# An attention and two-MLP kernel: the second MLP's Gelu writes back into its PSUM bank, and the cast and the subtraction read the bank instead of an SBUF tile

## The chip, the cores and the metric

The kernel runs on one core of one Trainium2 chip. The metric is device time in microseconds; it is given as the median of several runs. A profile is one execution recorded by the hardware profiler.

## The reference, cut to what matters

```python
# attention: q (1, 12288, 128); kv (1, 384, 32, 128), pooled over 4x4 windows -> 768 keys
kv_flat = kv_pool.reshape(B, -1, C) @ w_sr          # keys = values
a = softmax(q @ kv_flat.T / sqrt(C))
x = a @ kv_flat                                     # (12288, 128)
# first MLP, d_ff = 2048
h = x @ w_in;  g = maximum(h, 0) + alpha * minimum(h, 0);  y = g @ w_out
# second MLP, d_ff = 2048
h = y @ w_in2; g = h * (1 / (1 + exp(-1.702 * h)));        out = g @ w_out2
```

All arrays are float32. The second MLP's activation is the sigmoid form of Gelu, which ScalarE computes in one instruction (Gelu_apprx_sigmoid).

## The kernel before, in words

The tokens are cut into 24 tiles of 512 (TILES = 24, TOK = 512). The features (128) lie on the partitions, the tokens along the free dimension. Each product is done in float32r as three matmuls on operands that are split into a high part (a cast to float32r) and a low part (the exact value minus the high part): high x high, high x low, low x high (`passes`, L713 to L715, and L758, L761, L762 in `up`).

Each MLP has 2048 hidden features, in CH = 16 chunks of 128, numbered f. For every chunk:

- `up(t, m, f)` on TensorE (PE): three matmuls into bank f % 4 of the PSUM tile ps_h (RING = 4);
- first MLP (m = 0): `relu_hi` on ScalarE (ACT, L436) writes g_hi out of ps_h, and `relu_lo` on VectorE (DVE, L606) writes g_lo = relu(ps_h) - g_hi. Both read the bank;
- second MLP (m = 1): `gelu` on ACT (L440) reads ps_h and writes the SBUF tile g_full. The cast g_full to g_hi is made by ACT (L444) for odd f (CAST_ON_ACT) and by DVE (L614) for even f. `gelu_parts` on DVE then writes g_lo = g_full - g_hi (L616);
- `down(t, m, f)` on PE: three matmuls of g_hi and g_lo into ps_y1 or ps_y2. It waits on the semaphore g_split, which L606 and L616 increment.

PE runs `down(f - 3)` behind `up(f)` (LAG = 3). `up(f + 4)`, which fills the bank of f again, has no wait of its own: it stands behind `down(f)` in PE's order. In the second MLP of tile t the attention scores of tile t + 1 stand between up and down at f = 2, 4, 5, 7, 8 and 10 (SCORES_AT, ps_s); ACT copies them to s_sb (L419), DVE keeps a running maximum over them (`chunk_max`, L554), and behind f = 11 (MAX_AT) comes `token_max` (L560 to L580), which finds the maximum over the keys for each token and hands it to a DMA that spreads it over the partitions (max_row, max_sb). At f = 4 there is the split of the attention output (`attended_lo`, L621) and at f = 6 the inverse of the softmax's denominators (`inverse_sums`, L560 to L595). GpSimd (POOL) subtracts the maximum from the scores (L339) and sums the exponentials (L353). The first MLP of tile t holds the exponentials of tile t + 1 and the product with the values.

All orders are written out by hand, the same for each tile: tile 0, a hardware loop over tiles 1 to 21, then tile 22 (no scores and no maxima) and tile 23 (no attention at all). Every engine waits only on semaphores; a same-engine dependency has its own (act_done, dve_cast).

At the start g_full also serves as the place of the transposed first weight (w_in1T_sb), which one DMA of ACT's queue fills and which PE reads before the first Gelu (L824).

Of the kernel before, what the change touches and what calls it, by code (L numbers as in the profile page):

```python
# [11 lines left out]
P = 128  # L12
POOL = 4
WINDOW = POOL * POOL
TOK = 512
BLOCKS = TOK // P
LAG = 3
RING = 4
# [7 lines left out]
def attention_mlp_kernel(  # L26
# [14 lines left out]
    FF = w_in1.shape[1]  # L41
# [32 lines left out]
    with ExitStack() as ctx:  # L74
        def sb(name, shape, dt=F32):
            return ctx.enter_context(nc.sbuf_tensor(name, shape, dt))

        def psum(name, shape):
            return ctx.enter_context(nc.psum_tensor(name, shape, F32))

        def sem(name):
            return ctx.enter_context(nc.semaphore(name))

        ps_h = psum("ps_h", [P, RING, 512])
# [32 lines left out]
        y_lo = sb("y_lo", [P, TOK], F32R)  # L117
        g_hi = sb("g_hi", [P, RING, TOK], F32R)
        g_lo = sb("g_lo", [P, RING, TOK], F32R)
        g_full = sb("g_full", [P, RING, TOK])  # L120
        out_sb = sb("out_sb", [P, TOK])

        kv_raw = sb("kv_raw", [P, KV_RING, KV_KEYS, WINDOW])
# [16 lines left out]
        warm = sb("warm", [P, 1])  # L140
        warm_out = sb("warm_out", [P, 1])


        w_raw2 = kv_raw[:].rearrange("p r k w -> p (r k w)")
        w_in1T_sb = g_full[:].rearrange("p r n -> p (r n)")


        q0_raw, q0_hi, q0_lo = y_full, y_hi, y_lo
# [62 lines left out]
        act_cast = sem("act_cast")  # L211
        dve_cast = sem("dve_cast")
# [8 lines left out]
        def f32(ap):  # L221
            return ap.bitcast(F32)
# [27 lines left out]
        def casts_before(f, on_act):  # L250
            return sum((j in CAST_ON_ACT) == on_act for j in range(f))
# [141 lines left out]
        def _(act):  # L393
# [43 lines left out]

            def gelu(t, f):
                act.wait_ge(up_done, t * UPS + (CH + f + 1))
                nc.scalar.activation(g_full[:, f % RING, :], ps_h[:, f % RING, :],  # L440
                                     ACT.Gelu_apprx_sigmoid).then_inc(act_done, 1)
                if f in CAST_ON_ACT:
                    act.wait_ge(act_done, t * UPS + (CH + f + 1))
                    nc.scalar.copy(g_hi[:, f % RING, :], g_full[:, f % RING, :]).then_inc(act_cast, 1)  # L444

            def attended_hi(u):
                act.wait_ge(attended, u * KC + KC)
# [8 lines left out]
            def tile(t, attend, score):  # L456
                for f in range(LAG, CH):
                    relu_hi(t, f)
                    if attend and f in EXP_AT:
                        exponentials(t + 1, EXP_AT[f], t)  # L460
                        exponentials_hi(t + 1, EXP_AT[f])
                    if first(t) and f in W2_HI_AT:
                        second_hi(W2_HI_AT[f])
                nc.scalar.activation(warm_out[:], warm[:], ACT.Gelu_apprx_sigmoid)

                for f in range(CH):
                    gelu(t, f)
                    if score and f in SCORES_AT:
                        scores_to_sbuf(t + 1, SCORES_AT[f])
                    if attend and f == ATTENDED_AT:  # L470
                        attended_hi(t + 1)
                if attend:
                    nc.scalar.activation(warm_out[:], warm[:], ACT.Exp)
                    for f in range(LAG):
                        relu_hi(t + 1, f)

                act.wait_ge(y_complete, t * 2 + 2)
                if not first(t):
                    act.wait_ge(out_stored, t * DMA)
                nc.scalar.copy(out_sb[:], ps_y2[:]).then_inc(out_made, 1)  # L480
# [36 lines left out]
        def _(dve):  # L517
# [91 lines left out]
            def gelu_parts(t, f):  # L609
                if f in CAST_ON_ACT:  # L610
                    dve.wait_ge(act_cast, t * CASTS_ACT + (casts_before(f, True) + 1))
                else:
                    dve.wait_ge(act_done, t * UPS + (CH + f + 1))
                    nc.vector.tensor_copy(g_hi[:, f % RING, :], g_full[:, f % RING, :]).then_inc(dve_cast, 1)  # L614
                    dve.wait_ge(dve_cast, t * CASTS_DVE + (casts_before(f, False) + 1))
                nc.vector.tensor_tensor(g_lo[:, f % RING, :], g_full[:, f % RING, :], f32(g_hi[:, f % RING, :]),  # L616
                                        ALU.subtract).then_inc(g_split, 1)

            def attended_lo(u):
# [12 lines left out]
            def tile(t, attend, score):  # L632
                for f in range(LAG, CH):
                    relu_lo(t, f)
                    if score and f == QUERIES_AT:
                        queries_hi(t + 1)
                    if first(t) and f == FIRST_SUMS_AT:
                        inverse_sums(0)
                    if attend and f in LO_AT:
                        weights_lo(t + 1, LO_AT[f])  # L640
                for c in range(len(LO_AT), KC if attend else 0):
                    weights_lo(t + 1, c)

                divide(t)
                for f in range(CH):
                    gelu_parts(t, f)
                    if attend and f == ATTENDED_AT:
                        attended_lo(t + 1)
                    if attend and f == SUMS_AT:
                        inverse_sums(t + 1)  # L650
                    if score and SCORES_AT.get(f, 0) >= 1:
                        chunk_max(t + 1, SCORES_AT[f])
                    if score and f == MAX_AT:
                        token_max(t + 1)
                if attend:
                    for f in range(LAG):
                        relu_lo(t + 1, f)
# [211 lines left out]
```

## Time and profile before

| | |
|---|---|
| median of 3 runs | 1328.65 us (1327.99 to 1331.34) |
| profiled execution | 1329.05 us |
| its span in the profile | 1327.2 us, so 1.85 us lie around it |
| TensorE busy | 1288.1 us (97%) |
| VectorE busy | 992.1 us (75%) |
| ScalarE busy | 909.8 us (69%) |
| GpSimd busy | 409.5 us (31%) |
| mean granted TensorE clock | 0.993 of full speed |

The page gives busy time for each engine. Matmuls overlap in the engine, so a matmul's duration (about 390 ns) is longer than the distance from one start to the next (about 230 ns in the steady stretches). The times of DVE and ACT instructions overlap a little too: the next one can start before the record of the last one ends. The chain of work that ended last follows each instruction back to what released it.

### The profile page before, as it was taken

To read this page: it belongs to the slowest core of one execution; us is meant where nothing else is said; L and a number is where in the kernel's file an instruction comes from. 1 tells how busy PE (TensorE), PEld (TensorE's weight loads), DVE (VectorE), ACT (ScalarE), POOL (GpSimd) and SP (SyncE) were. 2 spreads that over 40 slices of the span, in tenths; PEclk is the share of its full clock that TensorE was granted. 3 is DMA by queue.
4 is the path that set the end of the run, shared out by engine and by line. 5 is a ranking of instruction groups with operands and counts; after the bars stand their busy time and mean duration, and the time that the engine had idled before them with its cause. 6 is when DMAs were issued, how large, how long until landed. Compare 5 with 4: busy or idle time off the path is not lost.

```text
span 1327.2 us, 18973 instructions
## 1 busy us (share of the span) xinstructions
PE 1288.1 (97%) x5608; PEld 1046.1 (79%) x5608; DVE 992.1 (75%) x1759; ACT 909.8 (69%) x1570; POOL 409.5 (31%) x305
## 2 busy tenths in 40 slices
PE   5689999999999999999999999999999999999998
PEld 3478888888888888888888888888888888888886
DVE  6997867768678677687786776877867768778665
ACT  3567667776776667767766677677666776776665
POOL 1773142241331422413314224133042241340400
PEclk9799999999999999999999999999999999999999
DMA  8201000000010000000100000000001000000000
GB/s 283 100 17 32 9 24 24 14 26 20 12 32 8 24 24 16 24 24 8 32 8 24 26 14 24 24 8 32 9 22 29 10 24 24 8 24 12 13 16 8
DMA packets 17935, 36.81 MB, mean 28 GB/s; under 512 B 3456, under 2 KB 3584, under 8 KB 17280
## 3 DMA queue, kind: packets, MB, share of 16 engines
q1 hardware_dynamic: 17488, 33.47, 7.8%
q10 hardware_dynamic: 432, 3.15, 0.6%
q8 instruction: 8, 0.13, 0.0%
q14 instruction: 7, 0.06, 0.0%
HBM read 30.22 MB, written 6.39 MB: 28 GB/s over the span
## 4 chain that ended last, share of the span: by engine, by line
PE 86%; DVE 10%; ACT 3%; issue 1%; DMA 1%; SPq 0%; POOL 0%; DVEq 0%; ACTq 0%
PE ps_y L713 13%; PE ps_y L714 12%; PE ps_y L715 12%; PE ps_h L761 12%; PE ps_h L762 12%; PE ps_h L758 11%; PE ps_x L713 2%; DVE g_lo L616 2%; PE ps_x L715 2%; PE ps_x L714 2%; PE ps_s L713 2%; PE ps_s L715 2%; PE ps_s L714 2%; DVE parts_max L562 1%; DVE pooled L560 1%; ACT g_full L440 1%
## 5 line engine op out<-in xcount | busy, mean ns | idle before, releaser
L606 DVE SCALAR_TENSOR_TENSOR g_lo<-ps_h,g_hi 128x512 fp32r<-128x512 f32 x384 | 262.8, 690 | 207.3 <-ACT g_hi L436 204.8
L339 POOL TENSOR_TENSOR s_sb<-s_sb,max_sb 128x512 f32<-128x512 f32 x138 | 174.5, 1301 | 655.2 <-DMA max_sb<-max_row 655.2
L440 ACT ACTIVATE g_full<-ps_h 128x512 f32<-128x512 f32 x384 | 229.7, 599 | 192.5 <-PE ps_h L762 181.5
L436 ACT ACTIVATE g_hi<-ps_h 128x512 fp32r<-128x512 f32 x384 | 227.1, 596 | 157.6 <-PE ps_h L762 157.1
L713 PE MATMUL ps_y<-g_hi,down_hi 128*128 128x512 f32 x768 | 302.1, 393 | 6.1 <-DVE g_lo L606 2.9
L714 PE MATMUL ps_y<-g_lo,down_hi 128*128 128x512 f32 x768 | 299.2, 390 | 0.0
L715 PE MATMUL ps_y<-g_hi,down_lo 128*128 128x512 f32 x768 | 299.1, 389 | 0.0
L616 DVE TENSOR_TENSOR g_lo<-g_full,g_hi 128x512 fp32r<-128x512 f32 x384 | 260.0, 688 | 38.3 <-ACT g_hi L444 31.7
L713 PEld LDWEIGHTS ps_y<-g_hi,down_hi 128*128 128x128 f32 x768 | 144.1, 188 | 46.6 <-DVE g_lo L616 12.4
L353 POOL TENSOR_TENSOR exp_sum<-exp_sum,s_sb 128x512 f32<-128x512 f32 x92 | 140.2, 1524 | 91.9 <-ACT s_sb L426 91.4
L715 PEld LDWEIGHTS ps_y<-g_hi,down_lo 128*128 128x128 f32 x768 | 144.2, 188 | 30.4
L714 PEld LDWEIGHTS ps_y<-g_lo,down_hi 128*128 128x128 f32 x768 | 144.2, 188 | 28.9
L761 PE MATMUL ps_h<-y_lo,up_hi 128*128 128x512 f32 x384 | 151.3, 394 | 0.9 <-DVE y_lo L630 0.9
L758 PE MATMUL ps_h<-y_hi,up_hi 128*128 128x512 f32 x384 | 149.6, 390 | 1.2 <-DVE y_hi L628 1.2
L758 PE MATMUL ps_h<-x_hi,up_hi 128*128 128x512 f32 x384 | 149.7, 390 | 0.0
L762 PE MATMUL ps_h<-y_hi,up_lo 128*128 128x512 f32 x384 | 149.7, 390 | 0.0
L761 PE MATMUL ps_h<-x_lo,up_hi 128*128 128x512 f32 x384 | 149.6, 390 | 0.0
L762 PE MATMUL ps_h<-x_hi,up_lo 128*128 128x512 f32 x384 | 149.4, 389 | 0.0
L444 ACT CAST g_hi<-g_full 128x512 fp32r<-128x512 f32 x192 | 119.4, 622 | 6.1
L601 DVE TENSOR_TENSOR a_lo<-s_sb,a_hi 128x512 fp32r<-128x512 f32 x138 | 113.0, 819 | 10.6 <-ACT a_hi L432 10.6
L614 DVE CAST g_hi<-g_full 128x512 fp32r<-128x512 f32 x192 | 81.2, 423 | 37.3 <-ACT g_full L440 35.2
L432 ACT CAST a_hi<-s_sb 128x512 fp32r<-128x512 f32 x138 | 86.0, 623 | 4.4
(142 smaller groups left out, 1714.4 us busy)
## 6 DMA issues: line engine op xcount, KB each, us to landing
kv_raw<-kvT SPq DMA_DIRECT2D x12, 512.0 KB, 5.5
inv_sb<-inv_row SPq DMA_DIRECT2D x24, 256.0 KB, 3.0
outT<-out_sb SPq DMA_DIRECT2D x24, 256.0 KB, 2.0
q_raw<-qT SPq DMA_DIRECT2D x23, 256.0 KB, 2.7
max_sb<-max_row SPq DMA_DIRECT2D x23, 256.0 KB, 3.1
w_raw<-w_in SPq DMA_DIRECT2D x1, 1024.0 KB, 8.0
w_raw<-w_out SPq DMA_DIRECT2D x1, 1024.0 KB, 9.9
g_full<-w_in1T ACTq DMA_DIRECT2D x1, 1024.0 KB, 5.2
```

Source lines behind the costliest of these rows:

```text
L339: nc.gpsimd.tensor_tensor(s_sb[:, c, :], s_sb[:, c, :], max_sb[:], ALU.subtract).then_inc(diff_done, 1)
L353: nc.gpsimd.tensor_tensor(exp_sum[:], (scores_of(u, 0) if c == 1 else exp_sum[:]), scores_of(u, c), ALU.add).then_inc(exp_sum_done, 1)
L436: nc.scalar.activation(g_hi[:, f % RING, :], ps_h[:, f % RING, :], ACT.Relu).then_inc(act_done, 1)
L440: nc.scalar.activation(g_full[:, f % RING, :], ps_h[:, f % RING, :], ACT.Gelu_apprx_sigmoid).then_inc(act_done, 1)
L606: nc.vector.scalar_tensor_tensor(g_lo[:, f % RING, :], ps_h[:, f % RING, :], 0.0, f32(g_hi[:, f % RING, :]), ALU.max, ALU.subtract).then_i ...
L616: nc.vector.tensor_tensor(g_lo[:, f % RING, :], g_full[:, f % RING, :], f32(g_hi[:, f % RING, :]), ALU.subtract).then_inc(g_split, 1)
L713: nc.tensor.matmul(out, w_hi_ap, m_hi_ap, start=start, stop=False)
L714: nc.tensor.matmul(out, w_hi_ap, m_lo_ap, start=False, stop=False)
L715: return nc.tensor.matmul(out, w_lo_ap, m_hi_ap, start=False, stop=stop)
L758: nc.tensor.matmul(ps_h[:, f % RING, :], up_hi[m][:, cols(f)], src_hi[:], start=True, stop=False)
L761: nc.tensor.matmul(ps_h[:, f % RING, :], up_hi[m][:, cols(f)], src_lo[:], start=False, stop=False)
L762: nc.tensor.matmul(ps_h[:, f % RING, :], up_lo[m][:, cols(f)], src_hi[:], start=False, stop=True).then_inc(up_done, 1)
```

## The change

Gelu writes its result back into the bank of ps_h from which it reads. The cast on ACT, the cast on DVE and DVE's subtraction read that bank. The SBUF tile g_full is given up, and w_in1T_sb gets a tile of its own of the same size. Semaphores, orders and loops stay as they are.

```diff
-        g_full = sb("g_full", [P, RING, TOK])
...
-        w_in1T_sb = g_full[:].rearrange("p r n -> p (r n)")
+        w_in1T_sb = sb("w_in1T_sb", [P, FF])[:]
...
             def gelu(t, f):
                 act.wait_ge(up_done, t * UPS + (CH + f + 1))
-                nc.scalar.activation(g_full[:, f % RING, :], ps_h[:, f % RING, :],
+
+                nc.scalar.activation(ps_h[:, f % RING, :], ps_h[:, f % RING, :],
                                      ACT.Gelu_apprx_sigmoid).then_inc(act_done, 1)
                 if f in CAST_ON_ACT:
                     act.wait_ge(act_done, t * UPS + (CH + f + 1))
-                    nc.scalar.copy(g_hi[:, f % RING, :], g_full[:, f % RING, :]).then_inc(act_cast, 1)
+                    nc.scalar.copy(g_hi[:, f % RING, :], ps_h[:, f % RING, :]).then_inc(act_cast, 1)
...
                     dve.wait_ge(act_done, t * UPS + (CH + f + 1))
-                    nc.vector.tensor_copy(g_hi[:, f % RING, :], g_full[:, f % RING, :]).then_inc(dve_cast, 1)
+                    nc.vector.tensor_copy(g_hi[:, f % RING, :], ps_h[:, f % RING, :]).then_inc(dve_cast, 1)
                     dve.wait_ge(dve_cast, t * CASTS_DVE + (casts_before(f, False) + 1))
-                nc.vector.tensor_tensor(g_lo[:, f % RING, :], g_full[:, f % RING, :], f32(g_hi[:, f % RING, :]),
+                nc.vector.tensor_tensor(g_lo[:, f % RING, :], ps_h[:, f % RING, :], f32(g_hi[:, f % RING, :]),
                                         ALU.subtract).then_inc(g_split, 1)
```

## Rows read from the trace of the kernel before

**Rows 1.** The page: busy us (share of the span) xinstructions of each engine

```profile
PE 1288.1 (97%) x5608; PEld 1046.1 (79%) x5608; DVE 992.1 (75%) x1759; ACT 909.8 (69%) x1570; POOL 409.5 (31%) x305
```

**Rows 2.** The chain in order of time: start us, us, engine, tile, line

```profile
107.25 0.61 ACT g_full L440
...
637.13 0.61 ACT g_full L440
...
642.67 0.50 PE ps_y L713
...
1220.13 0.61 ACT g_full L440
```

**Rows 3.** Timelines of ACT, DVE, PE, f = 6 and f = 11 to 12

```profile
628.21 0.60 ACT L440 ACTIVATE g_full<-ps_h 128x512 f32<-128x512 f32 x1 [0.30 <-PE ps_h L762]
...
628.84 0.43 DVE L614 CAST g_hi<-g_full 128x512 fp32r<-128x512 f32 x1
...
637.34 0.69 DVE L554 TENSOR_TENSOR running_max<-running_max,s_sb 128x512 f32<-128x512 f32 x1
638.42 0.69 DVE L616 TENSOR_TENSOR g_lo<-g_full,g_hi 128x512 fp32r<-128x512 f32 x1 [0.39 <-ACT g_hi L444]
...
641.92 1.29 DVE L616 TENSOR_TENSOR g_lo<-g_full,g_hi 128x512 fp32r<-128x512 f32 x2
...
645.86 1.29 DVE L606 SCALAR_TENSOR_TENSOR g_lo<-ps_h,g_hi 128x512 fp32r<-128x512 f32 x2 [0.98 <-ACT g_hi L436]
...
642.15 0.39 PE L762 MATMUL ps_h<-y_hi,up_lo 128*128 128x512 f32 x1
642.67 0.50 PE L713 MATMUL ps_y<-g_hi,down_hi 128*128 128x512 f32 x1
```

**Rows 4.** DVE's groups: operation, out<-in xcount | busy us, mean ns | idle before, releaser

```profile
L606 DVE SCALAR_TENSOR_TENSOR g_lo<-ps_h,g_hi 128x512 fp32r<-128x512 f32 x384 | 262.8, 690 | 207.3 <-ACT g_hi L436 204.8
L616 DVE TENSOR_TENSOR g_lo<-g_full,g_hi 128x512 fp32r<-128x512 f32 x384 | 260.0, 688 | 38.3 <-ACT g_hi L444 31.7
...
L614 DVE CAST g_hi<-g_full 128x512 fp32r<-128x512 f32 x192 | 81.2, 423 | 37.3 <-ACT g_full L440 35.2
...
L621 DVE TENSOR_TENSOR x_lo<-ps_x,x_hi 128x512 fp32r<-128x512 f32 x24 | 16.5, 689 | 1.7
...
L543 DVE TENSOR_REDUCE col_max<-ps_h 128x4 f32<-128x512 f32 x1 | 0.7, 691 | 0.2 <-PE ps_h L811 0.2
```

**Rows 5.** Timelines of DVE and PE: g_lo and down's matmul, f = 0 and 10

```profile
621.13 0.69 DVE L616 TENSOR_TENSOR g_lo<-g_full,g_hi 128x512 fp32r<-128x512 f32 x1
...
636.73 0.69 DVE L616 TENSOR_TENSOR g_lo<-g_full,g_hi 128x512 fp32r<-128x512 f32 x1
...
622.57 0.39 PE L713 MATMUL ps_y<-g_hi,down_hi 128*128 128x512 f32 x1
...
639.65 0.39 PE L713 MATMUL ps_y<-g_hi,down_hi 128*128 128x512 f32 x1
```

**Rows 6.** Timeline, f = 0 in tile 0 and in tile 22

```profile
90.29 1.41 DVE L614 CAST g_hi<-g_full 128x512 fp32r<-128x512 f32 x1 [1.45 <-ACT g_full L440]
...
92.58 0.47 PE L713 MATMUL ps_y<-g_hi,down_hi 128*128 128x512 f32 x1 [0.21 <-DVE g_lo L616]
...
1257.07 0.69 DVE L616 TENSOR_TENSOR g_lo<-g_full,g_hi 128x512 fp32r<-128x512 f32 x1
...
1257.91 0.47 PE L713 MATMUL ps_y<-g_hi,down_hi 128*128 128x512 f32 x1
```

**Rows 7.** Waits: who waited for whom: us in total, times, longest

```profile
POOL s_sb L339 <- DMA max_sb<-max_row: 655.2, 23, 30.4
```

**Rows 8.** ACT's groups, columns as in rows 4

```profile
L440 ACT ACTIVATE g_full<-ps_h 128x512 f32<-128x512 f32 x384 | 229.7, 599 | 192.5 <-PE ps_h L762 181.5
L436 ACT ACTIVATE g_hi<-ps_h 128x512 fp32r<-128x512 f32 x384 | 227.1, 596 | 157.6 <-PE ps_h L762 157.1
L444 ACT CAST g_hi<-g_full 128x512 fp32r<-128x512 f32 x192 | 119.4, 622 | 6.1
```

**Rows 9.** Stretch of one tile's second MLP: length, PE, PEld, DVE, ACT, POOL busy

```profile
619.08:647.60 28.52, 28.39 (x124) 22.85 (x123) 23.61 (x49) 21.03 (x36) 1.30 (x2) 1.00 0.07 19
```

## The prediction

> **What bounds the kernel now.** I read first the page's busy times: TensorE (PE) is busy 97% of the span, VectorE (DVE) 75%, ScalarE (ACT) 69% [rows 1]. So an engine other than PE costs time only where PE has to wait for it. Next I read the chain of work that ended last, in order of time, to find those places. In steady state it is PE matmuls one after another, and once a tile it leaves PE: the Gelu, cast and subtraction of f = 11, then DVE's row maximum (token_max), then the cast and subtraction of f = 12, and back to the matmul that reads them [rows 2]. The Gelu that opens this excursion stands 22 times in the chain, at 107.25 first and 1220.13 last, so a tile lasts (1220.13 - 107.25) / 21 = 52.99 us. The 22 are the tiles that call token_max (0 to 21 of 24). The reader is to see that from 637.13 to 642.67, 5.5 us of each tile's chain, the work is not PE's, and that the last link before PE is DVE.
>
> How much PE loses there is in the timeline. The L762 before the wait starts at 642.15; steady matmuls start 0.23 apart, so L713 of f = 12 was due at 642.38. It started at 642.67, 0.29 late and 0.06 after the g_lo of f = 12 ends (641.92 + 0.69 = 642.61) [rows 3]. From here on PE's start is the end of that g_lo plus 0.06: each nanosecond by which this g_lo comes later is a nanosecond of the tile.
>
> **The change, part by part.**
>
> *DVE's casts (L614), 192, eight a tile.* They now read PSUM instead of SBUF. The trace has no DVE cast or copy out of PSUM, so its cost is bounded. From below: 423 ns, as now. From above: DVE instructions over 128x512 with a PSUM input take 690 (L606), 689 (L621) and 691 (L543, whose only input is PSUM) [rows 4]. Nothing excludes either end. I take 690, so d = 0.267 us more for each cast, by nearness: all three that read PSUM agree within 2 ns, whatever their operation, and what sets the cheap L614 apart from them is that it has one input and that input is in SBUF, which is just what goes.
>
> The Trainium skill ("VectorE: DVE Perf Modes", sections "Mode 2×_2P — use both read ports for one tensor" and "Why PSUM operands drop a tier") says that a float32 copy doubles its rate by reading one tensor through both SBUF read ports, and that a float32 operand in PSUM holds it to the single rate. By that rule the sum is the one with d = 0.267; by the row of the cast alone it would be about nothing. No row of this trace shows such a cast.
>
> *Where these casts lie.* Going back from the g_lo of f = 12 at 641.92: DVE's only idle since the cast of f = 6 is the one before f = 11's g_lo at 638.42, which waited for ACT's cast. The instruction before it, L554 at 637.34, would have let it start 0.60 later (two g_lo in a row take 1.29, so the second starts 1.29 - 0.69 = 0.60 after the first), at 637.94: 0.48 us of slack. Before that DVE runs back to back to 628.84, where f = 6's cast waits for its Gelu (628.21 + 0.60) [rows 3]. The casts of f = 0, 2 and 4 have idle behind them before f = 6, and end there; the one nearest to the edge is f = 0, whose g_lo ends at 621.13 + 0.69 = 621.82 and whose matmul starts at 622.57, 0.75 of cover against 0.27 [rows 5]. So:
> - casts of f = 6, 8, 10: 3 x 0.267 = 0.80, less the slack of 0.48: f = 11's g_lo and token_max start 0.32 later;
> - cast of f = 12: 0.27 more, with no slack in front. The g_lo of f = 12 is 0.59 later, and so is PE.
> - The g_lo of f = 10, up to 0.80 later, ended at 636.73 + 0.69 = 637.42, and its matmul started at 639.65 [rows 5]: covered. So are f = 7 to 9, with less delay. Those from f = 13 on stand behind the stall, where PE is as late as they are.
>
> 22 tiles x 0.59 = 13.0 us. If the cover of 0.48 were gone, it would be 22 x 1.07 = 23.5.
>
> *The last two tiles and the first.* Tiles 22 and 23 have no scores and no maxima, so DVE has idle again; but the score matmuls in front of the first down are missing too. In tile 22 that matmul starts at 1257.91, right behind its g_lo (1257.07 + 0.69 = 1257.76) [rows 6]: no cover, 0.27 each, 0.5 us for both. In tile 0, f = 0's cast takes 1.41 us while POOL works, and its matmul starts at 92.58 instead of right after the three of up(3), at about 92.2 [rows 6]. If a cast out of PSUM isn't stretched by POOL, it takes 0.69, and 0.4 us come back. In later tiles POOL waits for max_sb's transfer during the second MLP (655.2 us in 23 waits [rows 7]), so there is no more of this kind.
>
> *DVE's subtractions (L616), 384.* One input from PSUM instead of SBUF: 688 now; the same operation with a PSUM input is L621, 689, and two L606 in a row take 1.29, as two L616 do [rows 3, 4]. Nothing.
>
> *ACT's casts (L444), 192.* 622 out of SBUF; the nearest out of PSUM is L436, 596 [rows 8]. 0.03 us less each, hidden: the wait for f = 11's cast, where it would count, is no longer the last to end.
>
> *ACT's Gelu (L440), 384.* Its destination becomes PSUM, and no row has ACT writing there. The nearest rows are the 622 and 596, where a source moved: 0.026. I take 0.02 less; bounds: 0.05 less and 0.05 more, twice that difference either way. It moves the point where f = 6's cast starts, so it counts once a tile: 22 x -0.02 = -0.4 us, between -1.1 and +1.1. The Trainium skill ("ScalarE: Activation LUTs", section "Step-by-step: what each stage is for") holds that ScalarE writes to PSUM faster than to SBUF; it would put the sum toward the -1.1, and no row here shows it.
>
> *Semaphores, ring, start.* No wait is added. Up(f + 4) stands behind down(f) on PE, and down(f) waits for g_lo, so each bank of ps_h was held that long already. The new tile for w_in1T is as large as the one given up, and its one transfer keeps its place in ACT's queue. Nothing.
>
> *Sum.* 13.0 + 0.5 - 0.4 - 0.4 = 12.7 us. The profiled execution took 1329.05 (span 1327.2 and 1.85 around it); its forecast is 1341.7. The median of the runs shown is 0.4 below it: 1341.3.
>
> **Rivals.**
> *The casts keep their rate, or DVE's 25% idle hides them.* For the first: their nearest row by operation is their own, 423. Against: the three PSUM readers. For the second the page's shares speak; the timeline doesn't allow it, since DVE can't run ahead of the Gelu of f = 6. Left are Gelu's -0.4 to -1.1 and tile 0's -0.4: 1327 to 1328, not slower. It decides where the cast stays under about 0.59: d = 0.17 gives 22 x (0.17 + 3 x 0.17 - 0.48) = 4.4 us. 10%.
> *Faster.* The casts stay, and ACT's pair (Gelu and cast, 599 + 622 [rows 8]) loses over 0.2 us together, so that f = 11's g_lo is earlier by that: 22 x 0.2 = 4.4 us, 1324. PE's lateness of 0.29 bounds it at 6.4 us. 3%.
> *Gelu into PSUM is dearer*, because ACT reads and writes one bank while PE fills the next. Each x us on a Gelu shifts f = 6 and so the tile: 22x on top. x = 0.26 gives 1347; from 0.47 on ACT fills the stage ((28.52 - 21.03) / 16 Gelus [rows 9]) and becomes the bound. No ACT row hints at it, none excludes it. 6%.
> *Reading PSUM costs DVE more for each instruction.* The most that rows allow is the 3 ns between L616 and L543: eleven instructions of the stretch from f = 6 to 12, 0.03 a tile, 0.7 us. The Trainium skill ("VectorE: DVE Perf Modes", section on the TRN2 errata) has 120 cycles of fixed cost for PSUM and 58 for SBUF at 0.96 GHz; by that an estimate of 0.065 on each of the eleven would make 0.7 a tile and 1357. The pairs of L606 speak against it. 2%.
>
> **How the numbers follow.** My forecast has 77%; its own range takes a cast of 0.68 to 0.70 (12.1 to 13.8 us instead of 13.0), Gelu's bounds and 1 us for the measurement: 1338 to 1345. A smaller loss whose reason I don't see, 1333 to 1337, has 2%. Within 0.3% (4 us, about what a measurement of this kernel tells from no change) is the first rival, 10%; faster 3%; slower 87%. The range of eight in ten takes in the dearer Gelu to x = 0.26 and part of the smaller loss: 1335 to 1347.
>
> **What would show it.** L614 near 690 ns with L616 still at 688; DVE's idle before f = 11's g_lo gone; L713 of f = 12 late by 0.88 instead of 0.29; tiles 53.6 us apart; the chain leaving PE at the Gelu of f = 6 instead of f = 11; tile 0's first cast short. The prediction is wrong if the casts stay under 0.59 us, if Gelu's mean is off 599 by over 50 ns, or if PE waits at more than one down a tile.

## The result, and the profile after

The changed kernel takes 1343.66 us (median of 4 runs, 1340.54 to 1344.53) against 1329.99 (4 runs, 1327.99 to 1331.89). The ratio is 1.0099, 95% interval 1.0074 to 1.0123: it is 13.7 us slower, and 1341.3 within 1335 to 1347 had been forecast. Its profiled execution took 1344.53 with a span of 1342.7, 15.5 us longer than the span of before.

From the page of the changed kernel: the span, and its busy line. Then its groups by line (columns as in rows 4); the code moved up by a line or two, so L613 is the old L614, L615 the old L616, L439 the old L440, L443 the old L444, L605 the old L606.

```profile
span 1342.7 us, 18973 instructions
PE 1290.8 (96%) x5608; PEld 1047.6 (78%) x5608; DVE 1038.9 (77%) x1759; ACT 900.0 (67%) x1570; POOL 409.2 (30%) x305
...
L439 ACT ACTIVATE ps_h<-ps_h 128x512 f32<-128x512 f32 x384 | 223.9, 583 | 203.0 <-PE ps_h L761 198.1
...
L615 DVE TENSOR_TENSOR g_lo<-ps_h,g_hi 128x512 fp32r<-128x512 f32 x384 | 257.2, 685 | 14.0 <-ACT g_hi L443 4.5
...
L613 DVE CAST g_hi<-ps_h 128x512 fp32r<-128x512 f32 x192 | 130.7, 681 | 37.8 <-ACT ps_h L439 34.5
...
L443 ACT CAST g_hi<-ps_h 128x512 fp32r<-128x512 f32 x192 | 112.8, 588 | 6.0
```

Four numbers answer to rows 4 and 8. DVE's cast went from 423 to 681 ns, its subtraction stayed (688 to 685), ACT's Gelu went from 599 to 583 and its cast from 622 to 588. DVE's busy time rose by 46.8 us in all, 49.5 of it from the 192 casts; the kernel lost 14. So most of the dearer casts is hidden, and the rest of the profile has to say where the others are not.

The chain of work that ended last, in order of time, in a window of the changed kernel (start us, us, engine, tile, line):

```profile
690.30 0.59 ACT ps_h L439
690.91 0.70 DVE g_hi L613
...
696.42 0.61 DVE g_hi L613
...
698.94 0.61 DVE g_hi L613
```

In rows 2 the chain left PE at the Gelu of f = 11. Now it leaves at the Gelu of f = 6 and follows DVE through the casts of f = 6, 8 and 10, inverse_sums and the chunk maxima, then through token_max and the cast and subtraction of f = 12: 15.0 us in which it is not PE's (636.74 to 651.73 in the tile below), against 5.5 before. Timelines of ACT, DVE and PE in the tile before this window show why (columns: start us, us, engine, line, operation, out<-in; in brackets the idle time in front and what ended it):

```profile
636.74 0.58 ACT L439 ACTIVATE ps_h<-ps_h 128x512 f32<-128x512 f32 x1 [0.35 <-PE ps_h L761]
...
646.28 0.59 ACT L443 CAST g_hi<-ps_h 128x512 fp32r<-128x512 f32 x1
...
637.36 0.69 DVE L613 CAST g_hi<-ps_h 128x512 fp32r<-128x512 f32 x1
...
646.63 0.68 DVE L553 TENSOR_TENSOR running_max<-running_max,s_sb 128x512 f32<-128x512 f32 x1
647.23 0.68 DVE L615 TENSOR_TENSOR g_lo<-ps_h,g_hi 128x512 fp32r<-128x512 f32 x1
...
650.30 0.65 DVE L613 CAST g_hi<-ps_h 128x512 fp32r<-128x512 f32 x1
650.99 1.29 DVE L615 TENSOR_TENSOR g_lo<-ps_h,g_hi 128x512 fp32r<-128x512 f32 x2
...
650.68 0.39 PE L761 MATMUL ps_h<-y_hi,up_lo 128*128 128x512 f32 x1
651.73 0.50 PE L712 MATMUL ps_y<-g_hi,down_hi 128*128 128x512 f32 x1 [0.67 <-DVE g_lo L615]
```

The idle of DVE in front of f = 11's g_lo (0.39 in rows 3) is gone: that g_lo starts at 647.23, 0.60 behind L553 and 0.36 behind the end of ACT's cast (646.28 + 0.59), so DVE itself is what it waits for. The g_lo of f = 12 ends at 650.99 + 0.69 = 651.68, PE's matmul starts 0.05 later; it was due at 650.68 + 0.23 = 650.91, so it is 0.82 late against 0.29 in rows 3: 0.53 more.

The waits say that no other wait of this kind joined in the steady tiles: PE's weight loads (PEld) behind the second MLP's g_lo in the kernel before, then PEld and PE in the changed one (us in total, times, longest). The count stays at 23, about one a tile, and the total goes up.

```profile
PEld ps_y L713 <- DVE g_lo L616: 12.4, 23, 0.6
```

```profile
PEld ps_y L712 <- DVE g_lo L615: 23.8, 23, 1.1
PE ps_y L712 <- DVE g_lo L615: 15.0, 24, 0.7
```

For the length of a tile the first division (y_full) of tile 1 and of tile 21 serve, 20 steady tiles apart. The changed kernel's two lines, then those of before:

```profile
144.16 0.69 DVE L625 TENSOR_TENSOR y_full<-ps_y,inv_sb 128x512 f32<-128x512 f32 x1 [0.38 <-PE ps_y L714]
...
1214.61 0.69 DVE L625 TENSOR_TENSOR y_full<-ps_y,inv_sb 128x512 f32<-128x512 f32 x1 [0.38 <-PE ps_y L714]
```

```profile
140.48 0.69 DVE L626 TENSOR_TENSOR y_full<-ps_y,inv_sb 128x512 f32<-128x512 f32 x1 [0.38 <-PE ps_y L715]
...
1200.34 0.69 DVE L626 TENSOR_TENSOR y_full<-ps_y,inv_sb 128x512 f32<-128x512 f32 x1 [0.38 <-PE ps_y L715]
```

(1214.61 - 144.16) / 20 = 53.52 us a tile against (1200.34 - 140.48) / 20 = 52.99: 0.53 more, as PE's lateness says. Tiles 1 to 21 together give 11.1 of the 15.5 us of span, tile 0 0.2, tile 22 0.5, tile 23 0.2. The other 3.5 lie in front of the first division (85.99 before, 89.45 after) and are not the change's: e7 below, which also has every Gelu in the bank, comes to its first division at 85.54 (see the last section).

### The profile page after: what moved, and what is told of

The parts are those of the page before. It is cut to its first block, busy times and chain, and to the rows that moved or that the text cites. A ratio compares the mean times of both kernels' runs of the same rounds, so it can differ in the third digit from the quotient of the medians.

```text
span 1342.7 us, 18973 instructions
## 1 busy us (share of the span) xinstructions
PE 1290.8 (96%) x5608; PEld 1047.6 (78%) x5608; DVE 1038.9 (77%) x1759; ACT 900.0 (67%) x1570; POOL 409.2 (30%) x305
## 4 chain that ended last, share of the span: by engine, by line
PE 70%; DVE 22%; issue 5%; ACT 2%; DMA 1%; SPq 0%; DVEq 0%; POOL 0%
PE ps_y L712 11%; PE ps_y L714 10%; PE ps_y L713 10%; PE ps_h L760 10%; PE ps_h L761 9%; PE ps_h L757 9%; DVE g_hi L613 4%; DVE g_lo L615 4%; DVE running_max L553 3%; PE ps_x L712 3%; PE ps_x L713 2%; PE ps_x L714 2%; DVE pooled L559 2%; DVE parts_sum L561 1%; DVE parts_max L561 1%
## 5 line engine op out<-in xcount | busy, mean ns | idle before, releaser
L605 DVE SCALAR_TENSOR_TENSOR g_lo<-ps_h,g_hi 128x512 fp32r<-128x512 f32 x384 | 264.8, 691 | 201.6 <-ACT g_hi L434 197.6
L439 ACT ACTIVATE ps_h<-ps_h 128x512 f32<-128x512 f32 x384 | 223.9, 583 | 203.0 <-PE ps_h L761 198.1
L712 PE MATMUL ps_y<-g_hi,down_hi 128*128 128x512 f32 x768 | 302.8, 394 | 18.4 <-DVE g_lo L615 15.0
L615 DVE TENSOR_TENSOR g_lo<-ps_h,g_hi 128x512 fp32r<-128x512 f32 x384 | 257.2, 685 | 14.0 <-ACT g_hi L443 4.5
L712 PEld LDWEIGHTS ps_y<-g_hi,down_hi 128*128 128x128 f32 x768 | 144.4, 188 | 60.0 <-DVE g_lo L615 23.8
L613 DVE CAST g_hi<-ps_h 128x512 fp32r<-128x512 f32 x192 | 130.7, 681 | 37.8 <-ACT ps_h L439 34.5
L443 ACT CAST g_hi<-ps_h 128x512 fp32r<-128x512 f32 x192 | 112.8, 588 | 6.0
```

The costliest lines, as they stand in the source:

```text
L439: nc.scalar.activation(ps_h[:, f % RING, :], ps_h[:, f % RING, :], ACT.Gelu_apprx_sigmoid).then_inc(act_done, 1)
L605: nc.vector.scalar_tensor_tensor(g_lo[:, f % RING, :], ps_h[:, f % RING, :], 0.0, f32(g_hi[:, f % RING, :]), ALU.max, ALU.subtract).then_i ...
L613: nc.vector.tensor_copy(g_hi[:, f % RING, :], ps_h[:, f % RING, :]).then_inc(dve_cast, 1)
L615: nc.vector.tensor_tensor(g_lo[:, f % RING, :], ps_h[:, f % RING, :], f32(g_hi[:, f % RING, :]), ALU.subtract).then_inc(g_split, 1)
L712: nc.tensor.matmul(out, w_hi_ap, m_hi_ap, start=start, stop=False)
```

## The experiments

Single executions of this kernel differ by some 4 us. So each experiment is read by the length of its steady tile, taken as above, beside its ratio to executions of the kernel before that ran together with it. How well that length repeats, two pairs show that should be equal: before and e5 (52.99 and 52.98), changed and e2 (53.52 and 53.53). The first five put only some chunks into the bank; g_full stays for the others:

```diff
+    IN_BANK = (1, 3, 5, 7, 9, 11, 13, 15)        # e1; the others: see each
...
+        def acts(f):
+            return (ps_h if f in IN_BANK else g_full)[:, f % RING, :]
...
-                nc.scalar.activation(g_full[:, f % RING, :], ps_h[:, f % RING, :],
+                nc.scalar.activation(acts(f), ps_h[:, f % RING, :],
...
-                    nc.scalar.copy(g_hi[:, f % RING, :], g_full[:, f % RING, :]).then_inc(act_cast, 1)
+                    nc.scalar.copy(g_hi[:, f % RING, :], acts(f)).then_inc(act_cast, 1)
```

and the same in DVE's cast and subtraction.

| kernel | divisions of tiles 1 and 21 at | a tile, us | median | ratio to before (interval) |
|---|---|---|---|---|
| before | 140.48, 1200.34 | 52.99 | 1329.99 | |
| changed | 144.16, 1214.61 | 53.52 | 1343.66 | 1.0099 (1.0074 to 1.0123) |
| e1, odd chunks in the bank | 143.62, 1201.14 | 52.88 | 1328.87 | 0.9991 (0.9981 to 1.0002) |
| e2, even chunks | 144.36, 1215.02 | 53.53 | 1344.59 | 1.0111 (1.0090 to 1.0131) |
| e3, f = 12 | 143.43, 1208.12 | 53.23 | 1334.39 | 1.0040 (1.0027 to 1.0054) |
| e4, f = 6, 8, 10 | 142.92, 1208.21 | 53.26 | 1337.78 | 1.0059 (1.0038 to 1.0080) |
| e5, f = 0, 2, 4 | 142.88, 1202.48 | 52.98 | 1331.30 | 1.0000 (0.9990 to 1.0009) |
| e6, before, f = 12's cast on ACT | 139.73, 1191.25 | 52.58 | 1320.62 | 0.9931 (0.9918 to 0.9944) |
| e7, changed, f = 12's cast on ACT | 139.31, 1195.26 | 52.80 | 1325.12 | 0.9960 (0.9947 to 0.9973) |
| e8, changed, all casts on ACT | 144.22, 1212.01 | 53.39 | 1341.12 | 1.0071 (1.0057 to 1.0084) |
| e9, e8 with the scores copied first | 139.41, 1192.10 | 52.63 | 1323.32 | 0.9956 (0.9940 to 0.9971) |
| e10, e6 with ACT's chunks in the bank | 139.97, 1190.64 | 52.53 | 1319.78 | 0.9930 (0.9916 to 0.9943) |

Medians are of each kernel's own runs (4 to 10); the kernel before that the ratios go by had medians of 1330.06 (e1 to e4), 1330.74 (e5 to e8) and 1329.70 (e9, e10). A tile's length comes from one profiled execution of each kernel.

**e1 and e2: is it the even casts or the bank?** For e2 IN_BANK is (0, 2, ..., 14).

> Only the odd chunks work in the bank (those whose cast ACT makes); the even ones keep g_full, so DVE's casts still read SBUF. Theory (the loss is DVE's even casts, dearer out of PSUM): casts stay at 423 ns, Gelu of odd chunks near 583 and ACT's cast near 588, f = 11's g_lo comes 0.05 us earlier, a tile lasts 52.94 us, the time is that of the kernel before less 1 us. Rival (working in the bank costs as such: ACT writing PSUM beside PE, more readers of it): half of the 0.53 us a tile, 53.26, 6 us slower than before.

> Only the even chunks work in the bank. Theory: the whole loss is here, casts near 681 ns, a tile lasts 53.52 us as in the changed kernel, 12 us slower than before. Rival (the bank as such): half, 53.26 us.

The whole loss is in e2, 0.54 us a tile; e1 is 0.11 shorter than before, though its whole time can't be told from before (0.9981 to 1.0002). The rival, that working in the bank costs as such, is refuted. e1's row of ACT's Gelu and cast by form (587 and 587 ns on average) shows the gain in place:

```profile
L444 ACT ACTIVATE ps_h<-ps_h 128x512 f32<-128x512 f32 x192 | 112.6, 587 | 98.0 <-PE ps_h L766 95.7
L448 ACT CAST g_hi<-ps_h 128x512 fp32r<-128x512 f32 x192 | 112.7, 587 | 6.0
```

It gained twice what had been expected (0.11, not 0.05). In e1 PE's matmul of f = 12 starts at 644.81, due 644.57 by the start of L766 at 644.34: 0.24 late, 0.05 less than in rows 3, as expected. Much of the rest is at another place: PE's weight loads for the scores waited for ACT's copy out of the one bank ps_s, 4.6 us in 22 waits before, 3.6 us in e1, 0.05 a tile. It was not isolated by a run of its own.

**e3, e4 and e5: which of the casts?** IN_BANK is (12,), (6, 8, 10) and (0, 2, 4).

> Only chunk f = 12 works in the bank: its cast stands right behind token_max with no slack. Theory: the cast's 681 - 423 = 0.258 us go into the tile whole, 53.25 us, 5.7 us slower. Rival (the loss is spread over the eight casts alike, one eighth each): 0.07 us, 53.06, 1.5 us slower.

> Only chunks f = 6, 8 and 10 work in the bank. Theory: 3 x 0.258 = 0.77 us, less the slack of 0.48 in front of f = 11's g_lo and 0.016 of the shorter Gelu: 0.28, a tile lasts 53.27 us, 6 us slower. Rival (no slack, they add in full): 53.75 us, 17 us slower. Rival (an eighth each): 0.2, 53.19.

> Only chunks f = 0, 2 and 4 work in the bank. Theory: DVE has idle behind each of them before f = 6, so a tile stays at 52.99 us; the two last tiles lose 0.27 each and tile 0 gets some tenths back, the time is that of before within 0.1%. Rival (an eighth of 0.53 each): 53.19 us, 4.4 us slower.

Measured are 53.23, 53.26 and 52.98 against the theory's 53.25, 53.27 and 52.99. One cast behind token_max costs as much (0.24) as three in front of it (0.27), since those share the slack of 0.48; three others cost nothing. The rivals of an eighth each (53.06, 53.19 and 53.19) and of no slack (53.75) are refuted. The parts add up: 0.24 + 0.27 + 0.00 = 0.51, beside 0.53 for the change.

**e6 and e7: is f = 12's cast the last link before PE?** One entry more in ACT's list, on the kernel before (e6) and on the changed one (e7):

```diff
-    CAST_ON_ACT = (1, 3, 5, 7, 9, 11, 13, 15)
+    CAST_ON_ACT = (1, 3, 5, 7, 9, 11, 12, 13, 15)
```

> The kernel before with the cast of f = 12 given to ACT (nine casts on ACT, seven on DVE), g_full kept. Theory (PE waits for the cast and the subtraction behind token_max and for nothing else in the steady tile): the g_lo of f = 12 starts at the end of token_max, 0.42 us earlier, and PE's wait of 0.29 with its restart of 0.1 goes: a tile lasts 52.6 us, 9 us faster than before. Rival (ACT's later Gelus and casts, or another chunk, become the wait): between 52.6 and 53.0.

> The changed kernel with the cast of f = 12 given to ACT. Theory: what is left of the delay is 3 x 0.258 - 0.48 = 0.29 at token_max, against 0.42 us of cast taken away in front of the g_lo: it starts 0.13 + 0.016 earlier than in the kernel before, PE waits 0.15 instead of 0.29, a tile lasts 52.8 us, 4 us faster than before, and 5 us slower than the kernel before with the same cast moved. Rival (the bank costs more than the casts): at or above 52.99.

52.58 and 52.80, as the theory had it. With this one cast moved, the kernel before gets 0.7% faster, and the changed one is faster than the original; between them stay 0.22 us a tile. In e7 the three casts have used up the slack, so PE still waits behind token_max: its L712 of f = 12 starts at 639.63 and was due at 639.23 + 0.23, 0.17 late against the 0.15 expected. The waits of e6 behind the second MLP's g_lo are down to two:

```profile
PEld ps_y L713 <- DVE g_lo L616: 0.8, 2, 0.5
```

The two kernels also run tile 0 at nearly the same times (first division at 85.67 and 85.54), with POOL summing exponentials at that moment in both. DVE's first cast of tile 0, out of SBUF in e6, and out of PSUM in e7:

```profile
89.96 1.42 DVE L614 CAST g_hi<-g_full 128x512 fp32r<-128x512 f32 x1 [1.45 <-ACT g_full L440]
```

```profile
89.82 0.69 DVE L613 CAST g_hi<-ps_h 128x512 fp32r<-128x512 f32 x1 [1.43 <-ACT ps_h L439]
```

So the cast out of SBUF is stretched beside POOL and the one out of PSUM is not. In e1, where POOL's sums end before it starts (93.71, then 94.02), the same cast out of SBUF takes 0.43. Tile 0 of e7 lasts 0.29 less than that of e6 (53.77 and 54.06 from division to division), although its steady tile lasts 0.22 more.

**e8: take all casts off DVE.**

```diff
-    CAST_ON_ACT = (1, 3, 5, 7, 9, 11, 13, 15)
+    CAST_ON_ACT = tuple(range(16))
```

> The changed kernel with all sixteen casts on ACT, none on DVE. Theory: DVE loses 8 x 0.68 us a tile and has idle again in front of f = 11, ACT gains 8 x 0.59 and is busy about 25 us of 28 in the second MLP; no down waits, a tile lasts 52.6 us, 9 us faster than before and 21 faster than the changed kernel. Rival (ACT becomes the bound, since Gelu, cast and the copy of scores take 1.6 us at six chunks): ACT back to back from f = 2 on and PE waiting at several chunks, above 53 us.

The theory failed: 53.39 us a tile. No down waits in a steady tile, but something else does:

```profile
PEld ps_s L712 <- ACT s_sb L417: 28.3, 66, 0.8
PE ps_s L712 <- ACT s_sb L417: 8.1, 22, 0.4
```

The score matmuls wait for ACT's copy of the scores before them, since ps_s is one bank. ACT's timeline in e8, around f = 4:

```profile
632.27 0.59 ACT L439 ACTIVATE ps_h<-ps_h 128x512 f32<-128x512 f32 x1
632.90 0.59 ACT L443 CAST g_hi<-ps_h 128x512 fp32r<-128x512 f32 x1
633.38 0.59 ACT L417 COPY s_sb<-ps_s 128x512 f32<-128x512 f32 x1
...
634.02 0.50 PE L712 MATMUL ps_s<-q_hi,k_hi 128*128 128x512 f32 x1 [0.37 <-ACT s_sb L417]
```

The new cast stands in front of the copy, and the matmul starts when the copy ends.

**e9: the same load on ACT in another order.** The cast is taken out of gelu and issued behind the copy:

```diff
                 for f in range(CH):
                     gelu(t, f)
                     if score and f in SCORES_AT:
                         scores_to_sbuf(t + 1, SCORES_AT[f])
+                    gelu_hi(t, f)
```

> The changed kernel with all casts on ACT, as in e8, but in the chunks that bring scores ACT copies the scores before it makes the cast. e8 had 53.39 us a tile, and its waits name the score matmuls, which waited for ACT's copy out of the one bank ps_s, not any down. Theory: the order on ACT is what cost, the casts themselves fit; the copies come as early as in the changed kernel, no down waits, a tile lasts 52.6 us, 9 us faster than the kernel before. Rival (ACT's load as such: 2 x 0.59 + 0.59 against two chunks' matmuls): 53 us or more again.

52.63: the order was the cost, not the load. The wait for the copy is down to 6.3 us in 22 waits. All sixteen casts read PSUM here, and the kernel is still faster than the original: it is DVE's casts that PSUM makes dear, not ACT's.

**e10: the bank where it pays.** IN_BANK and CAST_ON_ACT are both (1, 3, 5, 7, 9, 11, 12, 13, 15).

> Only the chunks whose cast ACT makes work in the bank, and f = 12 is one of them (1, 3, 5, 7, 9, 11, 12, 13, 15); DVE's seven casts read g_full in SBUF. Theory: the gains of e1 (ACT's Gelu and cast 0.05 shorter together, 0.02 us less wait of PE for the copy of scores) and of e6 (no wait behind token_max) add only in the second part: a tile lasts 52.5 to 52.6 us, 9 to 10.5 us faster than before, level with e6. Rival (the bank costs PE or DVE something that the stall hid so far): above e6's 52.58.

52.53, 0.05 below e6, at the better end of the expectation. Its time, 0.9930 of before, can't be told from e6's 0.9931. It is the shortest tile of all kernels run, with nothing lost to the bank.

## Why the prediction was right

- **The casts' price.** Taken as 690, measured 681 (423 before): d = 0.258 instead of 0.267. The choice between the two bounds was the whole sum, and it came out right. But the three rows of PSUM readers that it was taken from don't tell PSUM from SBUF: the subtraction takes 688 with both inputs in SBUF (L616) and 689 with one in PSUM (L621), and the reduction, which prediction and rows 4 show only out of PSUM (L543, 691), takes as long out of SBUF:

```profile
L562 DVE TENSOR_REDUCE parts_sum<-pooled 128x16 f32<-128x512 f32 x24 | 16.4, 685 | 0.8
```

So two of the three operations are as slow out of SBUF, and of the third (L606) there is no row out of SBUF. By the rows alone the choice of 690 was in part luck: only the changed kernel's row of 681 shows what a cast out of PSUM takes. The Trainium skill ("VectorE: DVE Perf Modes", section "Why PSUM operands drop a tier") says that a float32 operand in PSUM holds such a copy to the single rate, and this trace agrees (681 against 423).

- **Which casts count.** 0.80 less 0.48, plus 0.27: shown apart by e3, e4 and e5. With the measured d and Gelu (0.258 x 4 - 0.48 - 0.016) the step gives 0.536, measured 0.53 a tile. PE is 0.82 late at f = 12, where 0.88 had been forecast.
- **Subtractions.** Taken at nothing; 688 to 685.
- **ACT.** Gelu taken 0.02 shorter, 0.016 measured. The cast lost 0.034 and was called hidden. In the changed kernel it is; e1 shows that it is not where DVE's casts stay cheap, because ACT's cast of f = 11 then is a link of the chain.
- **Rivals.** "The casts keep their rate" fell with the row of 681. "Gelu into PSUM is dearer" fell with 583 and e1. "Reading PSUM costs DVE more for each instruction" fell with 685: the estimate of 0.065 us more from the figures of the Trainium skill ("VectorE: DVE Perf Modes", the section on the TRN2 errata) doesn't show in this kernel's subtractions. That DVE's idle hides the casts fell with e3 and e4, and "Faster" needed cheap casts.
- **The ends.** Tile 0 was to give 0.4 back; e6 and e7 show the mechanism (1.42 against 0.69). The profiled execution can't show it: it came to tile 0 late, and its first cast starts at 93.89, behind the end of POOL's sums at 93.59. That tile lost 0.2 instead of 0.53, and how much of this is the bank's is not shown. Tile 22 lost 0.47 instead of 0.27, and this is a miss of the reading: inverse_sums stands in tile 22 too, and the cast of f = 6 in front of it counts there: PE is late at a second down, by 0.34 (1282.88, due at 1282.54) against 0.10 before. e5 and e4 lose 0.24 and 0.26 in tile 22 (46.94 and 46.96 from division to division against 46.70), which together make it.
- **The sum.** 12.7 forecast; 12.0 for span without the start (15.5 - 3.5), 13.7 between the medians, 12.6 between the fastest executions (1340.54 and 1327.99).

## What to carry to other kernels

Before moving an operand to PSUM to save SBUF, look at which engine's single-input instructions read it: here DVE's float32 casts went from 423 to 681 ns, ACT's got 34 ns shorter, and DVE's two-input subtraction stayed. Work in the bank where ACT makes the cast, and keep DVE's casts in SBUF or give them to ACT (e10).

A cost on a busy engine counts from the last point where it waited, less the slack in front of the next one: walk back from the stall and add only those. The same walk finds the cheapest repair: one cast of sixteen moved (e6) gave some 9 us, and moving all of them (e8) lost that again to the order on the other engine.

## What the runs showed of the hardware that had not been expected

The profiled execution of the changed kernel had a lower granted clock of TensorE early on. Stretches 60 to 80 and 80 to 90 us: length, PE, PEld, DVE, ACT, POOL busy, granted clock, DMA share, GB/s. First the changed kernel, then before, then e1:

```profile
60.00:80.00 20.00, 16.77 (x70) 12.92 (x69) 18.51 (x27) 17.01 (x32) 18.85 (x14) 0.95 0.01 4
80.00:90.00 10.00, 10.00 (x36) 7.99 (x35) 8.13 (x10) 4.33 (x7) 6.04 (x5) 0.76 0.19 54
```

```profile
60.00:80.00 20.00, 17.14 (x76) 13.82 (x75) 19.40 (x28) 17.21 (x33) 18.13 (x14) 1.00 0.05 11
80.00:90.00 10.00, 9.32 (x42) 7.40 (x41) 8.48 (x11) 4.67 (x8) 9.47 (x6) 1.00 0.18 53
```

```profile
80.00:90.00 10.00, 10.00 (x35) 8.01 (x34) 7.99 (x10) 4.33 (x7) 6.04 (x5) 0.75 0.22 54
```

In it matmuls start 0.43 us apart until 84.6 us, at a granted clock of 0.50 (80 to 84 us), the lower of the two levels (1.2 GHz), and 0.23 behind it. In front of this PE had stood idle for 3.08 us; in the kernel before it had stood idle for 2.86 at the same place and kept a granted clock of 1.00. Up to 84.6 us neither kernel has run a Gelu of the second MLP, and e1, which loses nothing, has the same stretch at 0.75. It is a difference between executions, worth about 3.5 us here. Of the 17 executions of the kernel before that belong to e5 to e8, the ten with a mean granted clock of 0.993 or 0.994 took 1329.17 to 1330.75 us and the seven with 0.991 or 0.992 took 1331.69 to 1332.57, so the clock goes with much of the spread of single times; that it is the same stretch in them is not shown. What starts it was not tried.

That ACT's Gelu from PSUM to PSUM is 16 ns shorter than to SBUF (583 against 599; 12 ns within e1, which has both, 587 against 599), and its cast out of PSUM 34 ns shorter than out of SBUF (588 against 622), had been taken in direction but is now measured.
